# A fused attention and two feed-forward layers: v's first block by tokens, the constants as one row, smaller first loads

## The chip, the cores and the metric

The kernel runs on one core of a Trainium2 chip. Its engines are named as in the profile: PE (TensorE), DVE (VectorE), ACT (ScalarE), POOL (GpSimd) and SP (SyncE, which here only issues transfers). The metric is the device time of the kernel in microseconds (us); less is better.

## What is computed

Three stages in float32. The first is an attention over channels: the scores are a 256 x 256 matrix, and v is multiplied by their softmax.

```python
qn = q / (norm(q, axis=1) + 1e-6)                 # q, k, v: 6016 tokens x 256 channels
kn = k / (norm(k, axis=1) + 1e-6)
s = kn.T @ qn / tau
p = exp(s - s.max(-1));  p /= p.sum(-1) + 1e-9
x = v @ p                                          # 6016 x 256
h = x @ w_in                                       # 6016 x 2048
P = a[0] + a[1]*h + a[2]*h**2 + a[3]*h**3
Q = 1 + abs(b[0])*abs(h) + abs(b[1])*h**2
x = (P / (Q + 1e-6)) @ w_out                       # 6016 x 256
h = x @ w_in2
out = (h * clip(h + 3, 0, 6) / 6) @ w_out2         # 6016 x 256
```

## The kernel before, in words

Tokens are handled in tiles of 128 (47 of them, `TILES`), and behind the attention in blocks of four tiles (512 tokens; block 0 has three). C is 256 channels, F is 2048 hidden units, J = 16 chunks of 128 hidden units.

**Load stage.** q and k come in 24 loads (`loads`, line 65): tile 0 alone, then 23 pairs of tiles, in a ring of NQK = 8 buffers. SP issues them (lines 294 to 303), and from load 8 on it waits until the buffer has been multiplied by PE and squared by ACT. ACT issues k of load 0 itself (line 555). For each load PE adds k^T q into the PSUM tile OP (line 438; each product is four passes per tile), ACT squares q and k (line 574), and DVE adds the squares into square_sum (line 743). squares has two buffers, so ACT waits for DVE two loads back. Ahead of the first load PE runs `keep_clock(9)`, products of a matrix of ones.

**v and its transpose.** v is needed transposed. `load_v` (lines 285 to 292) brings a block in eight transfers, with runs of 32 channels (128 bytes), so that DVE's transpose of 32 x 32 squares (`v_transpose`, line 736) completes the transpose. For block 0 SP issues these eight after load 12 (`V0_LOADED`), and DVE transposes after load 14 (`V0_TRANSPOSED`). ACT rounds the result to the high half (`vT_split`, line 563), POOL subtracts for the low half (line 336). All products behind the attention take a high and a low half of each operand, as three passes (`split_product`, lines 405 to 407).

**Constants.** ACT issues three transfers that spread a, b and tau over all partitions (lines 556 to 558, 128 pieces each), and takes |b| and a square root of |b[1]| after load 2 (lines 576 to 580); DVE refines that root after load 3 (`exact_root`).

**Behind the loads.** After load 21 of 0 to 23 (`NORMS_BEHIND`) PE waits for `square_rows_summed` and sums the squares over the partitions (`norms`, line 419). ACT and DVE make inverse norms; PE spreads them after load 22 (`spread_inverse`, line 428). After load 23 DVE forms the logits (line 773), ACT their exponentials (line 594), PE transposes them (line 452). Then w_in1 is folded with them: `fold(n)` (line 465) gives two chunks of columns each, of which `fold_split` of ACT (line 604) and DVE (line 789) make halves; the first fold waits for the whole of w_in1 (line 454).

**Weights.** SP issues w_out1 in four parts (wd1), w_in1 in one transfer (line 306), v's block 1, w_in2 (wu2) and w_out2 (wd2) in four parts each. ACT rounds w_out1 (`wd1_round`, line 568) behind the loads, all four parts before the exponentials; POOL subtracts (`wd1_split`) once `square_rows_summed` is there; PE's `down1` waits for all four parts at its first chunk.

**Main part.** Step t has 16 slots j. In each slot, PE does `up2` and `down2` of the block before, `up1(t, j)`, and `down1` three chunks behind; ACT, DVE and POOL compute the gate functions in an order written out by hand in the `step` functions. In the first two steps, slots named in WU2_AT and WD2_AT also make the halves of w_in2 and w_out2. v's block t + 1 is transposed in slots 5 and 8. In step 0, `fold(n + 1)` comes behind `up1` of the chunk that uses fold n.

```python
LAG_DIVIDE = 1
LAG_DOWN1 = 3
...
V_AT = 5, 8
```

Of the kernel before, what the change touches and what calls it, by code (L numbers as in the profile page):

```python
# [26 lines left out]
P = 128  # L27


def attention_ffn_ffn(nc, q, k, v, tau, w_in1, w_out1, a, b, w_in2, w_out2, out):  # L30
# [25 lines left out]
    V0_LOADED, V0_TRANSPOSED = 12, 14  # L56

    NORMS_BEHIND, SPREAD_BEHIND = 21, 22
# [6 lines left out]
    loads = [(0, 1)] + [(i, min(QK, TILES - i)) for i in range(1, TILES, QK)]  # L65
    NQK = 8
    EPS_NORM, EPS_SUM, Q_CONST = 1e-6, 1e-9, 1.0 + 1e-6
# [3 lines left out]
    assert sum(PIECES) == J  # L71
# [17 lines left out]
    with ctx:  # L89
# [29 lines left out]
        v_blocks = sb("v_blocks", [P, CT, W], fp32)  # L119

# [34 lines left out]

        consts_in, qk_squared, qk_summed, qk_multiplied = map(
            sem, ("consts_in", "qk_squared", "qk_summed", "qk_multiplied"))
        qk_in = [sem(f"qk_in_{i}") for i in range(NQK)]
        w1_in, v_in = map(sem, ("w1_in", "v_in"))
# [111 lines left out]
        def _(sp):  # L271
# [3 lines left out]

            def load_wu2(part):
                half, c = part // 2, part % 2
                cols = slice(half * F // 2, (half + 1) * F // 2)
                sp.dma_start(wu2_raw[:, c, cols], w_up_h[1][:, c, cols]).then_inc(wu2_in[part], 16)
# [5 lines left out]
            def load_v(blk):  # L285
                m = width(blk) // P
                sp.wait_ge(vT_done, CT * blk)
                rows = tokens_of(v[0], blk, m).rearrange("(a q) (h b r) -> h b q a r", q=32, h=CT, b=4)
                to = v_blocks[:, :, 0:m * P].rearrange("p h (a r) -> p h a r", r=32)
                for c in range(CT):  # L290
                    for b in range(4):
                        sp.dma_start(to[32 * b:32 * (b + 1), c], rows[c, b]).then_inc(v_in, 16)

            for n, (i, m) in enumerate(loads):
                if n >= NQK:

                    sp.wait_ge(qk_multiplied, n - NQK + 1)
                    sp.wait_ge(qk_squared, n - NQK + 1)
                sp.dma_start(qk[:, n % NQK, 0, 0:m, :], q_h[:, i:i + m, :]).then_inc(qk_in[n % NQK], 16)
                if n >= 1:  # L300
                    sp.dma_start(qk[:, n % NQK, 1, 0:m, :], k_h[:, i:i + m, :]).then_inc(qk_in[n % NQK], 16)
                if n == V0_LOADED:
                    load_v(0)
            for part in range(4):
                load_wd1(part)
            sp.dma_start(w_raw_a[:], w_up_h[0]).then_inc(w1_in, 16)
            load_v(1)
            for part in range(4):
                load_wu2(part)
# [17 lines left out]
        def _(pool):  # L327
# [48 lines left out]
            for c in range(CT):  # L376
                vT_split(0, c, 0)

            pool.wait_ge(square_rows_summed, 1)
            for part in range(4):  # L380
                wd1_split(part)

            def step(t, par):
                for j in range(J):
                    if exists(t):
                        q_body(t, j)
                    if x := stage(t - 1, j - SHIFT2):
                        g2_split(*x)
                    if j in V_AT and exists(t) and exists(t + 1):
                        vT_split(t + 1, V_AT.index(j), 1 - par)  # L390
                    if slot(t, j) in WU2_AT:
                        wu2_split(WU2_AT.index(slot(t, j)))
                    if slot(t, j) in WD2_AT:
                        wd2_split(WD2_AT.index(slot(t, j)))
                    if y := stage(t, j - LAG_DIVIDE):
                        quotient_lo(*y)
# [5 lines left out]
        def _(pe):  # L402
# [30 lines left out]
            keep_clock(9)  # L433
            for n, (_, m) in enumerate(loads):
# [6 lines left out]
                done.then_inc(qk_multiplied, 1)  # L441
                if n == NORMS_BEHIND:
                    norms()
# [10 lines left out]
            pe.wait_ge(w1_in, 16)  # L454

            def fold(n):

                cols = columns(n)
                for c in range(CT):
# [23 lines left out]
            def down1(blk, j):  # L483
                w = width(blk)
                wait_chunk(pe, g1_lo_done, (blk, j))
                if j == 0 and isinstance(blk, int) and blk == 0:
                    pe.wait_ge(wd1_lo_done, 4)
# [64 lines left out]
        def _(act):  # L552

            _, m = loads[0]
            act.dma_start(qk[:, 0, 1, 0:m, :], k_h[:, 0:m, :]).then_inc(qk_in[0], 16)
            act.dma_start(coef[:, 0:4], a.partition_broadcast(P)).then_inc(consts_in, 16)
            act.dma_start(coef[:, 4:6], b.partition_broadcast(P)).then_inc(consts_in, 16)
            act.dma_start(coef[:, 6:7], tau.partition_broadcast(P)).then_inc(consts_in, 16)

            def vT_split(blk, c, par):  # L560
                w = width(blk)
                act.wait_ge(vT_done, CT * blk + c + 1)
# [7 lines left out]
            for n, (_, m) in enumerate(loads):  # L570
# [5 lines left out]
                if n == 2:  # L576
                    act.wait_ge(consts_in, 48)
# [3 lines left out]
                if n == V0_TRANSPOSED + 2:  # L581
                    for c in range(CT):
                        vT_split(0, c, 0)
# [6 lines left out]
            wd1_round(3)  # L590
# [90 lines left out]
            def step(t, par):  # L681
                for j in range(J):
# [15 lines left out]
                    if u2:  # L698
                        c2(*u2)
                    if slot(t, j) in WU2_AT:  # L700
                        wu2_round(WU2_AT.index(slot(t, j)))
# [9 lines left out]
        def _(dve):  # L711
# [18 lines left out]
            def v_transpose(blk, c, par):  # L730
                w = width(blk)
                if c == 0:
                    dve.wait_ge(v_in, 128 * (blk + 1))
# [5 lines left out]
            for n, (_, m) in enumerate(loads):  # L739
# [5 lines left out]
                if n == 3:  # L745
                    exact_root()
                if n == V0_TRANSPOSED:
                    for c in range(CT):
                        v_transpose(0, c, 0)
# [7 lines left out]
            dve.wait_ge(consts_in, 48)  # L757
# [135 lines left out]
```

## Time and profile before

| | us |
|---|---|
| runs shown (three) | 1155.82, 1157.50, 1157.81 |
| their median | 1157.5 |
| the profiled execution | 1158.11 |
| its span, first to last instruction | 1156.2 |
| PE busy in it | 1127.5 |
| DVE busy | 889.3 |
| ACT busy | 878.6 |
| POOL busy | 787.4 |

The span is the time between the first and the last instruction; the execution's own time is 1.9 us longer. The mean granted clock of PE is 0.992 of full speed. Busy times are sums over an engine's instructions. Four views are used below: the page, the chain of waits (from the last instruction back to what released each step), the instructions in order of time, with the idle time before each and what ended it in brackets, and stretches of fixed length with the busy time of each engine in them.

### The profile page before, as it was taken

How to read it: one execution, taken by the hardware profiler on the slowest of the kernel's cores; microseconds unless marked ns; L12 is line 12 of the kernel's file. 1: busy time of each engine (PE TensorE's matmuls, PEld its weight loads, DVE VectorE, ACT ScalarE, POOL GpSimd, SP SyncE). 2: the span in 40 equal slices, each digit the busy share in tenths (PEclk: the TensorE clock that was granted, in tenths of full speed). 3: DMA queues.
4: the chain of work that ended last, by engine and by line, in shares of the span. 5: the costliest groups of instructions: out<-in, count | busy, mean ns of one | idle time of the engine just before them, and what ended most of it. 6: DMA issues, size and time to landing. Idle time of an engine off the chain costs nothing.

```text
span 1156.2 us, 17900 instructions
## 1 busy us (share of the span) xinstructions
PE 1127.5 (98%) x6010; PEld 970.2 (84%) x6010; DVE 889.3 (77%) x1261; ACT 878.6 (76%) x1477; POOL 787.4 (68%) x628
## 2 busy tenths in 40 slices
PE   8988799999999999999999999999999999999998
PEld 7777588888888888888888888888888888888887
DVE  5679999887887887887787787787787788777621
ACT  5688888877877877777787787787787787787643
POOL 0458888776676676676676677677677677666643
PEclk9899899999999999999999999999999999999999
DMA  8951010010010010010010010010001000000000
GB/s 258 341 152 20 0 20 1 14 19 1 20 19 1 17 22 3 1 38 1 1 37 1 2 37 1 1 29 9 1 19 19 1 20 1 1 19 1 1 19 19
DMA packets 68378, 34.21 MB, mean 30 GB/s; under 512 B 51264, under 2 KB 61632, under 8 KB 68032
## 3 DMA queue, kind: packets, MB, share of 16 engines
q1 hardware_dynamic: 67712, 32.91, 10.3%
q8 instruction: 52, 0.85, 0.3%
q14 instruction: 38, 0.31, 0.1%
q10 hardware_dynamic: 576, 0.13, 0.1%
HBM read 26.87 MB, written 6.16 MB: 29 GB/s over the span
## 4 chain that ended last, share of the span: by engine, by line
PE 88%; DVE 6%; ACT 2%; issue 1%; DMA 1%; SPq 1%; POOL 0%; POOLq 0%; DVEq 0%; ACTq 0%
PE H L405 14%; PE H L406 14%; PE H L407 14%; PE OP L525 8%; PE OP L527 8%; PE OP L529 7%; PE YP L407 7%; PE YP L405 7%; PE YP L406 7%; DVE SQ L824 1%; DMA qk<-in_k 1%; PE OP L438 1%; DVE H L809 1%; DVE g_hi L817 1%; DVE square_sum L743 1%
## 5 line engine op out<-in xcount | busy, mean ns | idle before, releaser
L361 POOL TENSOR_TENSOR SQ<-SQ,AB 128x512 f32<-128x512 f32 (+1 forms) x192 | 248.0, 1292 | 283.4 <-ACT SQ L621 283.0
L373 POOL TENSOR_TENSOR g_lo<-R,g_hi 128x512 fp32r<-128x512 f32 (+1 forms) x192 | 245.1, 1276 | 30.6 <-ACT g_hi L652 30.6
L367 POOL TENSOR_TENSOR g_lo<-SQ,Y 128x512 fp32r<-128x512 f32 (+1 forms) x192 | 244.8, 1275 | 5.0 <-DVE SQ L832 5.0
L619 ACT ACTIVATE AB<-H,absb 128x512 f32<-128x512 f32 (+1 forms) x192 | 130.1, 678 | 151.2 <-PE H L407 150.0
L525 PE MATMUL OP<-wd_hi,g_hi 128*128 128x256 f32 x752 | 211.7, 282 | 0.6 <-POOL g_lo L373 0.6
L527 PE MATMUL OP<-wd_lo,g_hi 128*128 128x256 f32 x752 | 212.0, 282 | 0.0
L529 PE MATMUL OP<-wd_hi,g_lo 128*128 128x256 f32 x752 | 209.7, 279 | 0.0
L802 DVE TENSOR_TENSOR T<-T,H 128x512 f32<-128x512 f32 (+1 forms) x192 | 129.3, 674 | 103.9 <-ACT T L627 103.8
L817 DVE SCALAR_TENSOR_TENSOR g_hi<-H,coef,Y 128x512 fp32r<-128x512 f32 (+1 forms) x192 | 141.6, 738 | 68.3 <-ACT Y L640 67.3
L405 PE MATMUL H<-vT_hi,wf_hi 128*128 128x512 f32 (+1 forms) x384 | 151.3, 394 | 13.9 <-DVE wf_lo L789 8.1
L824 DVE SCALAR_TENSOR_TENSOR SQ<-SQ,g_hi 128x512 f32<-128x512 f32 (+1 forms) x192 | 155.4, 809 | 6.6
L646 ACT ACTIVATE R<-H 128x512 f32<-128x512 f32 (+1 forms) x192 | 113.2, 590 | 61.0 <-PE H L407 60.1
L838 DVE SCALAR_TENSOR_TENSOR R<-R,H 128x512 f32<-128x512 f32 (+1 forms) x192 | 128.2, 668 | 37.7 <-ACT R L646 37.7
L405 PE MATMUL YP<-g_hi,wd_hi 128*128 128x512 f32 (+1 forms) x384 | 151.5, 394 | 2.7 <-POOL g_lo L367 2.5
L405 PE MATMUL H<-yT_hi,wu_hi 128*128 128x512 f32 (+1 forms) x384 | 150.2, 391 | 0.7 <-issue 0.5
L406 PE MATMUL H<-vT_lo,wf_hi 128*128 128x512 f32 (+1 forms) x384 | 150.5, 392 | 0.0
L407 PE MATMUL H<-vT_hi,wf_lo 128*128 128x512 f32 (+1 forms) x384 | 150.4, 392 | 0.0
L407 PE MATMUL YP<-g_hi,wd_lo 128*128 128x512 f32 (+1 forms) x384 | 150.2, 391 | 0.0
L406 PE MATMUL H<-yT_lo,wu_hi 128*128 128x512 f32 (+1 forms) x384 | 149.7, 390 | 0.0
L406 PE MATMUL YP<-g_lo,wd_hi 128*128 128x512 f32 (+1 forms) x384 | 149.3, 389 | 0.0
L407 PE MATMUL H<-yT_hi,wu_lo 128*128 128x512 f32 (+1 forms) x384 | 149.0, 388 | 0.0
L525 PEld LDWEIGHTS OP<-wd_hi,g_hi 128*128 128x128 f32 x752 | 141.3, 188 | 8.8 <-POOL g_lo L373 0.8
(82 smaller groups left out, 2215.9 us busy)
## 6 DMA issues: line engine op xcount, KB each, us to landing
qk<-in_q SPq DMA_DIRECT2D x23, 256.0 KB, 5.4
qk<-in_k SPq DMA_DIRECT2D x23, 256.0 KB, 6.6
v_blocks<-in_v SPq DMA_DIRECT2D x88, 64.0 KB, 2.4
out<-o_tok SPq DMA_DIRECT2D x11, 512.0 KB, 3.0
wd_raw<-in_moe_w_out SPq DMA_DIRECT2D x8, 512.0 KB, 9.8
w_raw_a<-in_moe_w_in SPq DMA_DIRECT2D x1, 2048.0 KB, 13.6
wu_raw<-in_moe_w_in SPq DMA_DIRECT2D x4, 512.0 KB, 6.8
v_blocks<-in_v SPq DMA_DIRECT2D x8, 48.0 KB, 5.2
```

The source lines that it names most:

```text
L361: nc.gpsimd.tensor_tensor(SQ[:, j % 4, 0:w], SQ[:, j % 4, 0:w], AB[:, j % 2, 0:w], ALU.add)\
L367: nc.gpsimd.tensor_tensor(g1_lo[:, j % 4, 0:w], SQ[:, j % 4, 0:w], Y[:, j % 2, 0:w], ALU.mult)\
L373: nc.gpsimd.tensor_tensor(g2_lo[:, j % 4, 0:w], R[:, j % 2, 0:w], g2_hi[:, j % 4, 0:w].bitcast(fp32), ALU.subtract).then_inc(g2_lo_done, 1)
L405: nc.tensor.matmul(psum, w_hi, x_hi, start=first, stop=False)
L406: nc.tensor.matmul(psum, w_hi, x_lo, start=False, stop=False)
L407: return nc.tensor.matmul(psum, w_lo, x_hi, start=False, stop=last)
L525: nc.tensor.matmul(psum, g2_hi[:, j % 4, at], wd2_hi[:, j, :], start=first, stop=False, skip_group_check=True)
L527: nc.tensor.matmul(psum, g2_hi[:, j % 4, at], wd2_lo[:, j, :], start=False, stop=False, skip_group_check=True)
L529: done = nc.tensor.matmul(psum, g2_lo[:, j % 4, at], wd2_hi[:, j, :], start=False, stop=last, skip_group_check=True)
L619: nc.scalar.activation(AB[:, j % 2, 0:w], h, ACT.Abs, scale=absb[:, 0:1])
L817: nc.vector.scalar_tensor_tensor(g1_hi[:, j % 4, 0:w], h1(blk, j), A0, Y[:, j % 2, 0:w], ALU.add, ALU.mult).then_inc(g1_hi_done, 1)
L824: nc.vector.scalar_tensor_tensor(SQ[:, j % 4, 0:w], SQ[:, j % 4, 0:w], Q_CONST, g1_hi[:, j % 4, 0:w].bitcast(fp32), ALU.add, ALU.mult).the ...
```

## The change

- The first three tiles of q and k come as single loads, then 22 pairs: 25 loads. NORMS_BEHIND and SPREAD_BEHIND become 22 and 23, so they stand before the last two loads as they did. ACT issues k of loads 0 and 1. `keep_clock(9)` becomes `keep_clock(6)`.
- v's block 0 comes in one transfer, tokens on the partitions and 1 KB per token, after load 7. PE transposes it in six pieces after load 10, into the PSUM tile H; ACT copies the high halves and DVE subtracts for the low halves after load 14. POOL has no part in it.
- The constants come as one row on one partition, issued by ACT after its square of load 2. PE multiplies the row by a row of ones after load 6, which spreads it over the partitions; ACT copies it and takes |b| and the root after load 11, DVE refines the root after load 12.
- w_in1 comes in two halves of columns, behind parts 1 and 2 of w_out1; w_out1's part 3, w_in2's part 0 and v's block 1 follow. `fold` waits for the half that it needs.
- w_out1's part 3 is rounded and subtracted in slot 0 of step 0, and `down1` waits for each part where it needs it.

```diff
@@ settings @@
-    V0_LOADED, V0_TRANSPOSED = 12, 14
-    NORMS_BEHIND, SPREAD_BEHIND = 21, 22
+    V0_LOADED, V0_TRANSPOSED, V0_SPLIT = 7, 10, 14
+    COEF_SPREAD, COEF_USED = 6, 11
-    loads = [(0, 1)] + [(i, min(QK, TILES - i)) for i in range(1, TILES, QK)]
+    SINGLE = 3
+    loads = [(i, 1) for i in range(SINGLE)] + [(i, min(QK, TILES - i)) for i in range(SINGLE, TILES, QK)]
+    NORMS_BEHIND, SPREAD_BEHIND = len(loads) - 3, len(loads) - 2
@@ SP @@
+            def load_w1(half):
+                cols = slice(half * F // 2, (half + 1) * F // 2)
+                sp.dma_start(w_raw_a[:, :, cols], w_up_h[0][:, :, cols]).then_inc(w1_in[half], 16)
             def load_v(blk):
-                sp.wait_ge(vT_done, CT * blk)
+                if exists(blk - 2):
+                    sp.wait_ge(vT_done, CT * (blk - 1))
+                else:
+                    sp.wait_ge(vT_psum, CT)
...
-                if n >= 1:
+                if n >= 2:
                     sp.dma_start(qk[:, n % NQK, 1, 0:m, :], k_h[:, i:i + m, :]).then_inc(qk_in[n % NQK], 16)
                 if n == V0_LOADED:
-                    load_v(0)
-            for part in range(4):
-                load_wd1(part)
-            sp.dma_start(w_raw_a[:], w_up_h[0]).then_inc(w1_in, 16)
+                    m = tiles_of[0]
+                    sp.dma_start(v_tok[:, 0:m, :], tokens_of(v[0], 0, m).rearrange("(i p) c -> p i c", p=P))\
+                      .then_inc(v0_in, 16)
+            load_wd1(0)
+            load_wd1(1)
+            load_w1(0)
+            load_wd1(2)
+            load_w1(1)
+            load_wd1(3)
+            load_wu2(0)
             load_v(1)
-            for part in range(4):
+            for part in range(1, 4):
                 load_wu2(part)
@@ POOL @@
-            for c in range(CT):
-                vT_split(0, c, 0)
             pool.wait_ge(square_rows_summed, 1)
-            for part in range(4):
+            for part in range(3):
                 wd1_split(part)
...
+                    if slot(t, j) == 0:
+                        wd1_split(3)
@@ PE @@
-            keep_clock(9)
+            keep_clock(6)
...
+                if n == COEF_SPREAD:
+                    pe.wait_ge(consts_in, 48)
+                    nc.tensor.matmul(YP[:, 1, 0:7], ones[0:1, :], coef_row[:, 0:7], start=True, stop=True)\
+                      .then_inc(consts_spread, 1)
+                if n == V0_TRANSPOSED:
+                    pe.wait_ge(ident_ready, 1)
+                    pe.wait_ge(v0_in, 16)
+                    for c in range(CT):
+                        for i in range(tiles_of[0]):
+                            done = nc.tensor.transpose(H[:, c, i * P:(i + 1) * P], v_tok[:, i, c * P:(c + 1) * P],
+                                                       ident[:])
+                        done.then_inc(vT_psum, 1)
...
-            pe.wait_ge(w1_in, 16)
+                if PIECE_AT[n] in (0, J // 2):
+                    pe.wait_ge(w1_in[PIECE_AT[n] // (J // 2)], 16)
...
-                if j == 0 and isinstance(blk, int) and blk == 0:
-                    pe.wait_ge(wd1_lo_done, 4)
+                if j % 4 == 0 and isinstance(blk, int) and blk == 0:
+                    pe.wait_ge(wd1_lo_done, j // 4 + 1)
@@ ACT @@
-            _, m = loads[0]
-            act.dma_start(qk[:, 0, 1, 0:m, :], k_h[:, 0:m, :]).then_inc(qk_in[0], 16)
-            act.dma_start(coef[:, 0:4], a.partition_broadcast(P)).then_inc(consts_in, 16)
-            act.dma_start(coef[:, 4:6], b.partition_broadcast(P)).then_inc(consts_in, 16)
-            act.dma_start(coef[:, 6:7], tau.partition_broadcast(P)).then_inc(consts_in, 16)
+            for n, (i, m) in enumerate(loads[:2]):
+                act.dma_start(qk[:, n, 1, 0:m, :], k_h[:, i:i + m, :]).then_inc(qk_in[n], 16)
...
                 if n == 2:
-                    act.wait_ge(consts_in, 48)
+                    act.dma_start(coef_row[:, 0:4], a.rearrange("(o n) -> o n", o=1)).then_inc(consts_in, 16)
+                    act.dma_start(coef_row[:, 4:6], b.rearrange("(o n) -> o n", o=1)).then_inc(consts_in, 16)
+                    act.dma_start(coef_row[:, 6:7], tau.rearrange("(o n) -> o n", o=1)).then_inc(consts_in, 16)
+                if n == COEF_USED:
+                    act.wait_ge(consts_spread, 1)
+                    nc.scalar.activation(coef[:, 0:7], YP[:, 1, 0:7], ACT.Copy).then_inc(consts_ready, 1)
+                    act.wait_ge(consts_ready, 1)
                     nc.scalar.activation(absb[:], coef[:, 4:6], ACT.Abs).then_inc(absb_ready, 1)
...
-                if n == V0_TRANSPOSED + 2:
+                if n == V0_SPLIT:
+                    w = width(0)
                     for c in range(CT):
-                        vT_split(0, c, 0)
+                        act.wait_ge(vT_psum, c + 1)
+                        nc.scalar.activation(vT_hi[0][:, c, 0:w], H[:, c, 0:w], ACT.Copy).then_inc(vT_hi_done, 1)
...
-            wd1_round(3)
...
+                    if slot(t, j) == 0:
+                        wd1_round(3)
@@ DVE @@
-                if n == 3:
+                if n == COEF_USED + 1:
                     exact_root()
-                if n == V0_TRANSPOSED:
+                if n == V0_SPLIT:
+                    w = width(0)
                     for c in range(CT):
-                        v_transpose(0, c, 0)
+                        dve.wait_ge(vT_hi_done, c + 1)
+                        nc.vector.tensor_tensor(vT_lo[0][:, c, 0:w], H[:, c, 0:w], vT_hi[0][:, c, 0:w].bitcast(fp32),
+                                                ALU.subtract).then_inc(vT_lo_done, 1)
```

## Rows read from the trace of the kernel before

**Rows 1.** The page: busy time by engine, and the chain that ended last, by engine.

```profile
PE 1127.5 (98%) x6010; PEld 970.2 (84%) x6010; DVE 889.3 (77%) x1261; ACT 878.6 (76%) x1477; POOL 787.4 (68%) x628
...
PE 88%; DVE 6%; ACT 2%; issue 1%; DMA 1%; SPq 1%; POOL 0%; POOLq 0%; DVEq 0%; ACTq 0%
```

**Rows 2.** The chain of waits, 0 to 64 us (start us, us, what).

```profile
1.67 7.17 DMA qk<-in_k
...
47.60 0.70 DVE square_sum L751
...
50.22 3.62 PE OP L438 x8
53.84 0.85 PE YP L428 x4
...
56.72 0.50 DVE o_tok L773
```

**Rows 3.** Stretches of 1 us: busy of PE, PEld, DVE, ACT, POOL; PEclk, DMA share, GB/s.

```profile
18.00:19.00 1.00, 1.00 (x7) 0.87 (x6) 0.90 (x2) 0.73 (x2) 0.00 (x0) 1.00 1.06 395
...
24.00:25.00 1.00, 1.00 (x7) 0.87 (x6) 1.00 (x1) 1.00 (x1) 0.00 (x0) 1.00 0.47 69
...
48.00:49.00 1.00, 0.65 (x3) 0.65 (x4) 0.29 (x1) 0.20 (x1) 0.63 (x1) 0.56 1.18 413
...
55.00:56.00 1.00, 1.00 (x6) 0.89 (x5) 0.22 (x1) 0.00 (x0) 1.00 (x2) 1.00 0.65 66
```

**Rows 4.** In order of time, 0 to 30 us (start us, us, engine, line; [idle before]).

```profile
5.00 1.91 PE L438 MATMUL OP<-qk 128*128 128x256 f32 x4
...
8.89 21.35 PE L438 MATMUL OP<-qk 128*128 128x256 f32 x97 [1.97 <-DMA qk<-in_k]
...
10.48 1.06 ACT L574 ACTIVATE squares<-qk 128x1024 f32<-128x1024 f32 x1 [0.56 <-DMA qk<-in_k]
...
11.65 1.28 ACT L580 ACT_TABLE_LOAD   x1
...
16.94 8.57 SPq L292 DMA_DIRECT2D v_blocks<-in_v  x8
...
18.63 1.06 ACT L574 ACTIVATE squares<-qk 128x1024 f32<-128x1024 f32 x1 [0.27 <-DVE square_sum L743]
```

**Rows 5.** In order of time, 29 to 60 us, the same columns.

```profile
29.73 1.06 ACT L574 ACTIVATE squares<-qk 128x1024 f32<-128x1024 f32 x1 [3.40 <-DMA qk<-in_k]
29.75 15.91 PE L438 MATMUL OP<-qk 128*128 128x256 f32 x72
...
37.50 10.06 DVE L743 TENSOR_TENSOR square_sum<-square_sum,squares 128x1024 f32<-128x1024 f32 x7 [0.47 <-ACT squares L574]
...
45.97 2.23 ACT L568 ACTIVATE wd_hi<-wd_raw 128x1024 fp32r<-128x1024 f32 x2
...
48.35 1.87 PE L419 MATMUL YP<-ones,square_sum 128*128 128x1 f32 x8 [2.68 <-DVE square_sum L751]
48.37 9.28 POOL L336 TENSOR_TENSOR wd_lo<-wd_raw,wd_hi 128x1024 fp32r<-128x1024 f32 x4 [8.54 <-DVE square_sum L751]
...
56.45 1.50 PE L413 MATMUL H<-ones 128*128 128x128 f32 x12
```

**Rows 6.** DMA queues and issues, 0 to 12 us (KB each, us to landing).

```profile
q10 hardware_dynamic: 576, 0.13, 5.2%
...
coef<-in_tau ACTq DMA_DIRECT2D x1, 0.5 KB, 7.8
```

**Rows 7.** In order of time, DVE and POOL in the first slots.

```profile
65.05 0.56 DVE L802 TENSOR_TENSOR T<-T,H 128x384 f32<-128x384 f32 x1 [2.66 <-ACT T L627]
...
67.67 1.35 POOL L361 TENSOR_TENSOR SQ<-SQ,AB 128x384 f32<-128x384 f32 x1 [2.20 <-ACT SQ L621]
```

**Rows 8.** Stretches of 10 us and of 2 us, columns as in rows 3.

```profile
70.00:80.00 10.00, 8.02 (x43) 7.20 (x41) 9.29 (x18) 9.27 (x21) 7.29 (x7) 1.00 0.30 96
...
124.00:126.00 2.00, 0.00 (x0) 0.00 (x0) 1.88 (x3) 1.87 (x4) 1.95 (x3) 0.50 0.00 0
```

More of the change, by code:

```diff
@@ L70, in attention_ffn_ffn @@
     PIECE_AT = [sum(PIECES[:i]) for i in range(len(PIECES))]
-    assert sum(PIECES) == J
+    assert sum(PIECES) == J and J // 2 in PIECE_AT
     QUARTER, UNIT = J * C // 4, J * C // 8
@@ L119, in attention_ffn_ffn @@
         v_blocks = sb("v_blocks", [P, CT, W], fp32)
+        v_tok = v_blocks[:].rearrange("p h w -> p (h w)").rearrange("p (i c) -> p i c", c=C)
+        coef_row = sb("coef_row", [1, 8], fp32)
         o_tok = sb("o_tok", [P, BT, C], fp32)
@@ L153, in attention_ffn_ffn @@
         A0, A1, A2, A3, B0, B1, TAU = (coef[:, i:i + 1] for i in range(7))
+        consts_ready = sem("consts_ready")
         consts_in, qk_squared, qk_summed, qk_multiplied = map(
@@ L158, in attention_ffn_ffn @@
         qk_in = [sem(f"qk_in_{i}") for i in range(NQK)]
-        w1_in, v_in = map(sem, ("w1_in", "v_in"))
+        w1_in = [sem(f"w1_in_{i}") for i in range(2)]
+        v0_in, v_in, vT_psum, consts_spread = map(sem, ("v0_in", "v_in", "vT_psum", "consts_spread"))
         wd1_in, wu2_in, wd2_in = ([sem(f"{x}_in_{i}") for i in range(4)] for x in ("wd1", "wu2", "wd2"))
@@ L552, in _ @@
         def _(act):
-            _, m = loads[0]
-            act.dma_start(qk[:, 0, 1, 0:m, :], k_h[:, 0:m, :]).then_inc(qk_in[0], 16)
-            act.dma_start(coef[:, 0:4], a.partition_broadcast(P)).then_inc(consts_in, 16)
-            act.dma_start(coef[:, 4:6], b.partition_broadcast(P)).then_inc(consts_in, 16)
-            act.dma_start(coef[:, 6:7], tau.partition_broadcast(P)).then_inc(consts_in, 16)
+            for n, (i, m) in enumerate(loads[:2]):
+                act.dma_start(qk[:, n, 1, 0:m, :], k_h[:, i:i + m, :]).then_inc(qk_in[n], 16)
             def vT_split(blk, c, par):
                 w = width(blk)
-                act.wait_ge(vT_done, CT * blk + c + 1)
+                act.wait_ge(vT_done, CT * (blk - 1) + c + 1)
                 nc.scalar.activation(vT_hi[par][:, c, 0:w], vT_raw[par][:, c, 0:w], ACT.Copy).then_inc(vT_hi_done, 1)
@@ L732, in v_transpose @@
                 if c == 0:
-                    dve.wait_ge(v_in, 128 * (blk + 1))
+                    dve.wait_ge(v_in, 128 * blk)
                     if exists(blk - 2):
@@ L756, in _ @@
             ratio, norm, norm_k = small[:, 12:16], YP[:, 0, 8:12], small[:, 16:18]
-            dve.wait_ge(consts_in, 48)
+            dve.wait_ge(consts_ready, 1)
             dve.wait_ge(roots_taken, 1)
```

## The prediction

> **What bounds the kernel now.** I read the page first: PE is busy 98% of the span and carries 88% of the chain that ended last [rows 1]. From about 140 us on, time is matmul time, which this change does not touch. What can be won lies in the start, where an earlier finish moves everything behind it one for one. So I read the start in the chain of waits, then in stretches of 1 us, then in order of time.
>
> PE computes the product of k and q until 45.7 us and then waits for DVE's sum of squares: the fold of its two halves starts at 47.60 [rows 2], the norms' matmuls at 48.35, after 2.68 us of idle PE [rows 5]. Then come norms, load 22, the spread of the inverses and load 23, until DVE takes the logits at 56.72 [rows 2]. The granted clock falls at 48 and is back at 1.00 by 55 [rows 3]; between, PE runs at 1.2 of 2.4 GHz, and load 22 took 3.62 us [rows 2] for what takes 1.73 at full clock.
>
> Why is DVE late? Eight v issues (L292) hold SP for 8.57 us from 16.94 [rows 4]. DMA falls from 395 to 69 GB/s [rows 3], and ACT and DVE run dry near 27 us: the wait of ACT that ends at 29.73 took 3.40 us [rows 5]. Otherwise DVE is the pace: 7 adds in 10.06 us [rows 5] include waits, and where nothing is late ACT starts a square each 1.33 us, 1.06 of work and 0.27 of waiting for DVE [rows 4]. PE hardly notices the hole (its passes run on from 8.89 to 45.66, broken off only near 29.75): those 42 tiles in 36.8 us [rows 4, 5], allowing 0.5 for gaps, give 0.863 per tile, 1.73 per pair, more than a pair's 1.33 on DMA or DVE. PE is the slowest of the three in the load stage, yet DVE comes last.
>
> **The change, part by part.**
>
> *Start of the load stage.* Tile 0 runs from 5.00 to 6.91 at 0.48 us a pass, half speed, then PE idles 1.97 until the pair of tiles 1 and 2 has landed; the next pair came at 10.48 [rows 4]. With single tiles and 12 warm-up passes instead of 18, tile 0 starts near 3.9 and tiles 1 and 2 fit into the wait. After that PE needs load 3 (tiles 3 and 4, the old load 2). Bounds for it: 10.45 as now, and 7.6, when PE would be through with tiles 0 to 2 at full speed. The constants' packets (most of the 576 on ACT's queue; tau took 7.8 us to land [rows 6]) lie among the first tiles and now go as three short rows. I take 9.4, nearer the old row, as the queue still starts slowly. Load 1's k now goes by ACT's queue. It landed 7.17 us after its issue began [rows 2], and an issue is under 0.5, so issuing is not what was late. The Trainium skill, "DMA: Bandwidth & Descriptors", section "Issuing engines are not separate DMA queues", says that a second issuing engine saves only the time of issuing. By it the pair would come at most 0.5 us sooner, 9.95, and the total gain would be 0.55 smaller; the range holds that.
>
> *v's first block.* SP's eight issues become one of about 0.45 us for 384 KB, 1.0 us of DMA at 390 GB/s. PE gets six 128x128 transposes: 0.75 at the warm-up's pace of 12 passes in 1.50 [rows 5], 1.3 at the pace of the 4 passes of the spread, 0.85 [rows 2]; I take 1.0, between. PE now waits for v at load 10, with all later matmuls behind it. It is issued after load 7, near 12 us; with even 7.2 us to land it is there by 20, PE at 9.4 + 8 x 1.73 = 23: no wait. POOL loses two subtractions that nobody waited for: 0. DVE loses its two transposes and gets two subtractions of 0.56 (its 128x384 form from PSUM [rows 7]), 1.15 with waits; ACT copies ahead of it.
>
> *Constants.* 0.2 us of PE behind load 6 (there at 16.3). ACT issues the rows after its third square, near 8 us, three at 0.45, before load 3 is needed. If the last took 7.8 us as now it lands by 17.3: 0 to 1 us of PE wait; I take 0, since a single row is less than 128. The work on them (copy, abs, table load 1.28 [rows 4], root: 1.75 us) moves from load 2 to load 11, where ACT leads DVE by only 0.27 + 0.24: DVE starves 1.24 us, plus 0.78 for the exact root that it computes.
>
> *DVE's new end.* Squares of load 3 done at 10.5; 22 pairs at 1.33, 29.3; 1.24 + 0.78 + 1.15; fold 0.7: 43.7. *PE's new end of load 22*: 9.4 + 20 x 1.73 + 1.0 + 0.2 = 45.2. So PE no longer waits: norms at 45.3 instead of 48.35. SP must wait for PE before load 24 (buffer of load 16 free at 35); it lands by 41, ahead of both.
>
> *Behind the sum.* PE arrives without an idle stretch, so I let the clock stay up: norms 1.0 (1.87 at half [rows 5]), pair 1.73, spread 0.5, pair 1.73, hand-over 0.1: logits at 50.4 instead of 56.72, **6.3 us sooner**. The inverses take ACT and DVE 1.5 us, inside the pair's 1.73. On ACT, rounds 0 and 1 of w_out1 (landed by 42) are done by 46, round 2 and the exp table by 50. w_in1's first half lands near 45, its second near 49, and the first fold comes at 53: halving it gives 0 here, costs 0.5 us of SP.
>
> *What is given back.* Round 3 of w_out1 (half of 2.23 [rows 5], 1.0 us) moves from an idle ACT into slot 0, ahead of the next root; POOL's part (a quarter of 9.28 [rows 5]) falls where POOL idled 2.20 for ACT [rows 7]. ACT has no gap there, so its 1.0 is lost whole, plus 0 to 1 from POOL running beside DVE; I take **1.2**. The split wait on w_out1: 0, all parts were there. v block 1 is issued about 2 us earlier and needed at slot 5: 0. w_in2's first part lands before slot 2: 0.
>
> **Sum:** -6.3 + 1.2 = -5.1 us. The profiled execution took 1158.1 (span 1156.2), so 1153.0; the median of the three runs shown, 1157.5, gives 1152.4. I say 1152.6, between, as the three differ by 2.0 among themselves.
>
> **The rivals.**
> (a) *The sum of squares is late again.* For: two stalls of ACT and DVE now lie in steady state, and adds at 1.33 never catch up. Against: the v hole (3.4) goes, and DVE leads by 1.5. Ready at 46.5, it costs 1.2: 1153.8. Ready at 48, the clock falls as it did, and only some 0.4 of the stage and none of its low clock is won; with 1.2 given back, 1158.3, no change. Between them 1156. Chance 0.09.
> (b) *The clock falls in the first slots*, where PE idles 1 us more. PE was busy 8.02 of 10 us from 70 to 80 at clock 1.00 [rows 8]; at half clock that is 16, so 10 us of it do the work of 6.2 and cost 3.8: 1156.4, no change. For: the clock was 0.50 at 124 to 126, where PE stood still [rows 8]. Against: idle stretches between slots are one us, not five. Chance 0.06.
> (c) *Slower: PE stays at half clock in the load stage.* Six fewer warm-up passes, and waits between single tiles. Each pair so run costs 1.73 more and nothing hides it, since PE is the pace. Three pairs cancel the gain; from 4.3 (until about 24 us) it is slower by over 0.2%; six give 1163.0. For: half speed lasted from the first pass to past 6.9. Against: at 8.89, after 1.97 us of waiting, it was gone [rows 4], and the waits are now shorter. The Trainium skill, "TensorE: Matmul & The Clock Gate", section "What's actually happening", says that throttled is the default and activity releases it; by that, less warm-up speaks for this rival. Tiles 1 and 2 replace it, however. Chance 0.04.
> (d) *The change does not do what it says*: DMA thins out after load 7 for a reason other than SP's eight issues. DVE then ends near 46.7, PE waits 1.5: 1154.1. Chance 0.05.
> Forecast: 0.76.
>
> **How the numbers follow.** 0.2% is 2.3 us, about what a measurement of this kernel can tell from no change, so faster means below 1155.2. Forecast, (d) and a third of (a) are faster; the rest of (a) and (b) no change; (c) slower: 0.84, 0.12, 0.04. Bounds of the terms: load 3 at 7.6 leaves DVE's 43.7 to decide, -1.5; slot 0 without loss, -1.2; load 3 as now +1.05, constants late +1, POOL +0.8, and PE's low clock near 124 may last 0.5 longer or shorter. Not all at once: 1150.2 to 1155.8, with (d) and the mild (a) inside.
>
> **What would show it.** Right: no thin DMA at 22 to 28; PE without a gap from load 3 to the norms, whose wait for square_sum is gone; clock 1.00 from 45 to 60; logits near 50.4; a slot 1 about 1 us later against slot 0. Wrong: PE waits for constants or v; a clock of 0.5 before 60; a pair at 3.4 us after 8 us; norms still near 48.

## The result, and the profile after

The changed kernel takes 1141.47 us (median of four runs, 1141.41 to 1142.12), the kernel before 1157.51 (1155.82 to 1157.81): the ratio is 0.9866, with a 95% interval of 0.9849 to 0.9883. Forecast were 1152.6, at most 1155.8 and at least 1150.2. The sign was right, the gain was 16.0 us instead of 4.9, and the range missed it by 9 us.

The page after (busy time by engine; the chain by engine), beside [rows 1]:

```profile
PE 1112.6 (98%) x6012; PEld 960.9 (84%) x6012; DVE 889.3 (78%) x1262; ACT 878.9 (77%) x1479; POOL 782.6 (69%) x626
...
PE 91%; DVE 5%; ACT 2%; issue 1%; DMA 0%; POOL 0%; SPq 0%; POOLq 0%; DVEq 0%; ACTq 0%
```

PE is busy for 14.9 us less, though it has two passes more to do. Up to the logits it is busy for 51.6 us before and 47.6 after; most of that is the low clock behind the loads. From the first output copy to the end it has 5032 instructions in both kernels and is busy for 928.4 us before and 918.2 after. These 10.2 us are new; the prediction has no term for them.

The chain of waits at the start (start us, us, what), beside [rows 2]:

```profile
8.19 7.17 PE OP L459 x32
...
44.15 0.79 PE YP L440 x8
44.94 1.83 PE OP L459 x8
46.77 0.48 PE YP L449 x4
...
49.09 0.49 DVE o_tok L816
```

The wait for square_sum is gone from the chain. PE goes from the loads straight into the norms; the load behind the norms takes 1.83 us instead of 3.62, and DVE has the logits at 49.09 instead of 56.72. Stretches of 1 us (length, busy of PE, PEld, DVE, ACT, POOL; PEclk, DMA share, GB/s), beside [rows 3]:

```profile
24.00:25.00 1.00, 1.00 (x7) 0.87 (x6) 1.00 (x1) 0.85 (x1) 0.00 (x0) 1.00 1.05 383
...
48.00:49.00 1.00, 1.00 (x7) 0.90 (x6) 0.00 (x0) 0.98 (x2) 0.45 (x1) 1.00 1.09 380
55.00:56.00 1.00, 1.00 (x6) 0.95 (x6) 0.00 (x0) 0.99 (x3) 0.00 (x0) 1.00 0.67 106
```

DMA moves 383 GB/s at 24 us where it moved 69, and the clock stays at 1.00. In order of time, beside [rows 4]:

```profile
3.76 2.23 PE L459 MATMUL OP<-qk 128*128 128x256 f32 x8
...
6.36 1.13 PE L459 MATMUL OP<-qk 128*128 128x256 f32 x4 [0.36 <-DMA qk<-in_k]
...
7.96 0.51 SPq L319 DMA_DIRECT2D v_blocks<-in_v  x1
8.16 1.06 ACT L605 ACTIVATE squares<-qk 128x1024 f32<-128x1024 f32 x1 [1.20 <-DMA qk<-in_k]
...
22.61 0.82 PE L472 MATMUL H<-ident,v_blocks 128*128 128x128 f32 x6
```

v goes out in one issue of 0.51 us. Tiles 3 and 4 have landed at 8.16 instead of 10.48. The six transposes take 0.66 us of PE by the chain. Behind the loads, beside [rows 5, 7]:

```profile
42.41 0.69 DVE L794 TENSOR_TENSOR square_sum<-square_sum 128x512 f32<-128x512 f32 x1
...
43.99 0.95 PE L440 MATMUL YP<-ones,square_sum 128*128 128x1 f32 x8
...
55.71 0.58 ACT L657 ACTIVATE AB<-H,absb 128x384 f32<-128x384 f32 x1
...
57.20 1.07 ACT L599 ACTIVATE wd_hi<-wd_raw 128x1024 fp32r<-128x1024 f32 x1
...
58.35 2.39 POOL L357 TENSOR_TENSOR wd_lo<-wd_raw,wd_hi 128x1024 fp32r<-128x1024 f32 x1 [0.50 <-ACT wd_hi L599]
...
59.87 0.56 ACT L657 ACTIVATE AB<-H,absb 128x384 f32<-128x384 f32 x1
```

DVE's fold starts at 42.41 and the norms at 43.99, about 0.9 us after it ends. Round 3 of w_out1 sits in slot 0 (57.20), POOL's part behind it (58.35). From AB of slot 0 to AB of slot 1 it is 4.16 us; it was 63.34 to 66.55, 3.21. So the start keeps 7.63 - 0.95, some 6.7 us. ACT's copy of the first block's output starts at 215.71 instead of 222.08: 6.4 us sooner.

**Where the other 10 us are.** The spans differ by 16.6 us (1156.2 and 1139.6), so 10.2 come behind the first output. The copies of the later blocks drift apart, block by block. ACT's copies of two successive outputs, before and then after:

```profile
849.79 1.01 ACT L667 ACTIVATE o_tok<-OP 128x1024 f32<-128x1024 f32 x1
...
939.29 1.01 ACT L667 ACTIVATE o_tok<-OP 128x1024 f32<-128x1024 f32 x1
```

```profile
836.23 1.01 ACT L705 ACTIVATE o_tok<-OP 128x1024 f32<-128x1024 f32 x1
...
924.77 1.01 ACT L705 ACTIVATE o_tok<-OP 128x1024 f32<-128x1024 f32 x1
```

A block takes 89.50 us before and 88.54 after; between most of its neighbours it is the same to 0.02 us. Yet PE is never idle there, and its clock is 1.00 in both (20 us of each, columns as above, before and then after):

```profile
900.00:920.00 20.00, 20.00 (x106) 16.98 (x105) 14.87 (x21) 14.80 (x26) 12.91 (x11) 1.00 0.00 1
```

```profile
900.00:920.00 20.00, 20.00 (x112) 17.28 (x112) 16.50 (x24) 15.92 (x28) 14.79 (x12) 1.00 0.01 1
```

PE's own instructions start at shorter distances. The profile models the end of a matmul, so the starts are compared. The first of the twelve passes of the second down product in a slot, and the instruction behind the twelve, before and after:

```profile
903.84 0.28 PE L525 MATMUL OP<-wd_hi,g_hi 128*128 128x256 f32 x1
...
905.26 0.40 PE L405 MATMUL H<-vT_hi,wf_hi 128*128 128x512 f32 x1
```

```profile
900.75 0.28 PE L559 MATMUL OP<-wd_hi,g_hi 128*128 128x256 f32 x1
...
902.12 0.40 PE L426 MATMUL H<-vT_hi,wf_hi 128*128 128x512 f32 x1
```

Twelve passes take 1.42 us before and 1.37 after. Over three whole blocks, the passes of the second down product follow each other every 118.3 ns before and 114.7 after, and the 512-column passes every 231.9 and 230.9. With 192 and 288 of them in a block that is 0.68 + 0.28 = 0.96 us. The passes of the loop are the same. What differs is that the new tensor coef_row (its declaration is not in the cut diff above) takes 32 bytes per partition behind v_blocks, so o_tok, yT, R, g2, T, SQ, AB, Y and g1 lie 32 bytes further on, while weights and v lie where they were.

### The profile page after: what moved, and what is told of

The parts are those of the page before. It is cut to its first block, busy times and chain, and to the rows that moved or that the text cites. A ratio compares the mean times of both kernels' runs of the same rounds, so it can differ in the third digit from the quotient of the medians.

```text
span 1139.6 us, 17909 instructions
## 1 busy us (share of the span) xinstructions
PE 1112.6 (98%) x6012; PEld 960.9 (84%) x6012; DVE 889.3 (78%) x1262; ACT 878.9 (77%) x1479; POOL 782.6 (69%) x626
## 3 DMA queue, kind: packets, MB, share of 16 engines
q1 hardware_dynamic: 65328, 32.78, 10.2%
## 4 chain that ended last, share of the span: by engine, by line
PE 91%; DVE 5%; ACT 2%; issue 1%; DMA 0%; POOL 0%; SPq 0%; POOLq 0%; DVEq 0%; ACTq 0%
PE H L426 15%; PE H L428 14%; PE H L427 14%; PE OP L559 7%; PE OP L563 7%; PE OP L561 7%; PE YP L426 7%; PE YP L428 7%; PE YP L427 7%; PE OP L459 3%; DVE SQ L867 1%; DVE H L852 1%; DVE g_hi L860 1%; DVE T L845 1%; DMA qk<-in_k 0%
## 5 line engine op out<-in xcount | busy, mean ns | idle before, releaser
L559 PE MATMUL OP<-wd_hi,g_hi 128*128 128x256 f32 x752 | 209.2, 278 | 0.6 <-POOL g_lo L394 0.6
L563 PE MATMUL OP<-wd_hi,g_lo 128*128 128x256 f32 x752 | 209.0, 278 | 0.0
L561 PE MATMUL OP<-wd_lo,g_hi 128*128 128x256 f32 x752 | 208.9, 278 | 0.0
L852 DVE SCALAR_TENSOR_TENSOR H<-T,coef,H 128x512 f32<-128x512 f32 (+1 forms) x192 | 143.0, 745 | 6.7
L561 PEld LDWEIGHTS OP<-wd_lo,g_hi 128*128 128x128 f32 x752 | 141.2, 188 | 8.2
```

The source lines that it names most:

```text
L559: nc.tensor.matmul(psum, g2_hi[:, j % 4, at], wd2_hi[:, j, :], start=first, stop=False, skip_group_check=True)
L561: nc.tensor.matmul(psum, g2_hi[:, j % 4, at], wd2_lo[:, j, :], start=False, stop=False, skip_group_check=True)
L563: done = nc.tensor.matmul(psum, g2_lo[:, j % 4, at], wd2_hi[:, j, :], start=False, stop=last, skip_group_check=True)
L852: nc.vector.scalar_tensor_tensor(h, T[:, j % 2, 0:w], A1, h, ALU.add, ALU.mult).then_inc(t3_done, 1)
```

## The experiments

Eighteen kernels ran. Block times are the distance of ACT's output copies in the second half of the loop; for the kernels with a single run the block time is what is read. Each ratio is to the kernel before, on the same chip, with its 95% interval. The chip is not the same for all experiments, and the kernel before had medians of 1157.3 to 1159.0 us on them.

**The shift alone, and the change without it.** pad32 is the kernel before with an unused tensor; row_in_small is the changed kernel with the row in spare columns.

```diff
 v_blocks = sb("v_blocks", [P, CT, W], fp32)
+sb("pad", [P, 8], fp32)                        # pad32
...
-coef_row = sb("coef_row", [1, 8], fp32)
+coef_row = small[0:1, 41:48]                   # row_in_small
```

> The kernel before, with one unused tensor of 32 bytes per partition behind v_blocks and nothing else, so that o_tok, yT, R, g2, T, SQ, AB, Y and g1 lie where they lie in the changed kernel (yT_hi at byte 158144 instead of 158112, a multiple of 64). The changed kernel's blocks in the long loop take 88.53 us each, those of before 89.49, with PE never idle in either. Theory A (where the tensors lie sets PE's pace): 88.5 us a block and about 1147 us in all, the start as before (logits at 56.7). Rival B (the program, its waits or the start set the pace): 89.5 a block and 1157.5.

> The changed kernel, with the row of constants in seven unused columns of the tensor small, so that no tensor is moved against the kernel before. Theory A: blocks of 89.5 us, about 1152 us in all, the start as in the changed kernel (logits at 49.1). Rival B: 88.5 us a block and 1141.5.

pad32: 1146.77 us, ratio 0.9897 (0.9873 to 0.9920), with this pair of copies, 88.53 us apart:

```profile
841.68 1.01 ACT L668 ACTIVATE o_tok<-OP 128x1024 f32<-128x1024 f32 x1
...
930.21 1.01 ACT L668 ACTIVATE o_tok<-OP 128x1024 f32<-128x1024 f32 x1
```

row_in_small: 1151.81 us, ratio 0.9943 (0.9924 to 0.9961), blocks of 89.49, logits at 48.56. The kernel before had a median of 1158.2 us on that chip. Theory A holds in both directions: 32 unused bytes are worth 11.4 us by themselves, and the change without them is worth 6.4, which is inside the forecast. The logits of pad32 came at 55.66, where 56.7 was expected; the paragraph on place or distance shows why.

**Other distances.** The same padding with 64, 96, 160, 480 and 544 bytes.

> The kernel before with 64 unused bytes at the same place: the tensors move, but they start 32 bytes past a multiple of 64 as before. Theory A in its sharp form (the remainder by 64 decides): 89.5 us a block and 1157.5. If the address matters in another way (the distance between tensors before and behind the padding, or a larger unit), anything between 88.5 and 90 a block.

> The kernel before with 96 unused bytes at the same place: yT_hi at byte 158208, a multiple of 128. Sharp form of theory A (remainder by 64): as with 32 bytes, 88.5 us a block and 1147. If the remainder by 128 also counts (the changed kernel's is 64), it is faster than with 32 bytes.

> The kernel before with 160 unused bytes behind v_blocks: the back is at remainder 64 by 128 again, but 128 bytes further than with 32. If the pattern repeats every 128 bytes: 88.5 us a block and 1147. If it is longer than 128 or no pattern of this kind at all: another block time, 89.5 or more.

> The kernel before with 544 = 512 + 32 unused bytes behind v_blocks. With 32 the blocks take 88.53 us, with 160 = 128 + 32 they take 89.60. If the pattern of places repeats with 512 bytes (or 256): 88.53 a block. If not, 89.5 or more, and what counts is no remainder by a small power of two.

> The kernel before with 480 unused bytes behind v_blocks, by 512 the step of 32 bytes to the other side. No theory of mine gives the number: 88.5 us a block would say that several places are fast, 89.5 or more that the fast one stands alone among the six tried.

| bytes behind v_blocks | block, us | kernel, us | ratio (95%) |
|---|---|---|---|
| 0 (before) | 89.49 | 1157.5 | |
| 32 | 88.53 | 1146.8 | 0.9897 (0.9873 to 0.9920) |
| 64 | 89.60 | 1159.0 | 1.0008 (0.9995 to 1.0020) |
| 96 | 89.81 | 1159.6 | 1.0010 (0.9998 to 1.0022) |
| 160 | 89.60 | 1158.6 | 0.9999 (0.9989 to 1.0009) |
| 480 | 88.64 | 1147.9 | one run |
| 544 | 88.53 | 1148.1 | one run |

The copies with 96 bytes, 89.81 apart:

```profile
850.52 1.01 ACT L668 ACTIVATE o_tok<-OP 128x1024 f32<-128x1024 f32 x1
...
940.33 1.01 ACT L668 ACTIVATE o_tok<-OP 128x1024 f32<-128x1024 f32 x1
```

The sharp form of theory A fell: with 96 bytes the tensors start at a multiple of 64, and of 128, and their blocks are longer than before. A pattern of 128 fell with 160 bytes. 544 = 512 + 32 gives the block time of 32, so a pattern of 512 (or 256) fits. 480 is a second fast place, with another mix of passes (119 ns for the second down product, 226 to 227 for the 512-column passes that read yT or g1).

**Place or distance.** both_moved puts 64 bytes in front of all tensors and 32 behind v_blocks; all_moved puts 32 in front of all and none behind.

```diff
+sb("pad_a", [P, 16], fp32)    # both_moved; [P, 8] in all_moved
 wf_hi, wf_lo = (sb(f"wf_{x}", [P, CT, F], f32r) for x in ("hi", "lo"))
...
 v_blocks = sb("v_blocks", [P, CT, W], fp32)
+sb("pad_b", [P, 8], fp32)     # both_moved alone
```

> Remainders by 128 of the start bytes, in the four kernels so far: weights and v (in front) 0; yT, R, g2, T, SQ, AB, Y, g1 (behind) 32, 64, 96 and 0 for 0, 32, 64 and 96 bytes of padding, and only 64 was fast. Here 64 unused bytes stand in front of all and 32 behind v_blocks: the front lies at 64 and the back at 0. Theory A1 (what counts is how front and back lie to each other, 64 apart is fast): 88.5 us a block, 1147. Theory A2 (the place of the back tensors alone counts): as with 96 bytes, whose back lies at the very same bytes, 89.8 a block and 1159.

> The kernel before with 32 unused bytes in front of all tensors: the back at the very bytes of the fast kernels, but the front (weights, v) moved as well. Theory A1 (how front and back lie to each other): 89.49 us a block. Theory A2 (the place of the back itself): 88.53.

both_moved: blocks of 88.53, 1144.66 us, ratio 0.9882 (0.9863 to 0.9902), with its back tensors at the very bytes at which pad96 is slow. all_moved: blocks of 89.49, 1158.5 us in its one run, with its back tensors at the bytes of the fast kernels. So the place itself does not decide. The distance between what lies in front (weights, v) and behind (yT, g2, g1) does.

both_moved is also 2 us ahead of pad32 at the start: its logits come at 53.65 instead of 55.66. Most of that is the granted clock, as the norms start at 48.45 and 48.81. The stretch of 2 us behind the norms, both_moved and then pad32 (columns as above):

```profile
50.00:52.00 2.00, 2.00 (x13) 1.70 (x12) 1.21 (x8) 1.98 (x3) 2.00 (x2) 1.00 1.02 434
```

```profile
50.00:52.00 2.00, 2.00 (x6) 1.60 (x6) 1.29 (x8) 1.98 (x4) 2.00 (x2) 0.53 0.98 410
```

Thirteen of the profiled kernels have the start of the kernel before. Behind the idle time in front of the norms the clock was at half for about 7 us in five of them (the kernel before is one), for about 3.5 us in seven, and not at all in both_moved; their logits came between 53.65 and 58.17. The start of a single profile can therefore not be compared to a microsecond, while block times at equal distances agree within 0.02 us.

**Whose tensors.** Two trials, g2_only and all_but_g2, were made before the pattern was known. They restored places by steps of 128 bytes, which pad160 shows not to be neutral.

```diff
+sb("pad_a", [P, 8], fp32)     # g2_only; [P, 24] in all_but_g2, with [P, 8] behind v_blocks
 g2_hi, g2_lo = (sb(f"g2_{x}", [P, 4, W], f32r) for x in ("hi", "lo"))
+sb("pad_b", [P, 24], fp32)    # [P, 8] in all_but_g2
```

> The kernel before with 32 unused bytes in front of g2_hi and 96 behind g2_lo: g2 (the stationary operand of the second down product) alone stands at remainder 64, the rest of the back at 32 as before. The passes that have g2 start every 118.2 ns before and every 114.7 in the changed kernel; 192 of them a block are 0.67 of the 0.96 us. Theory A3 (the place of g2 itself counts for them): 114.7 ns, 88.8 us a block, near 1151. Rival (they are slow through traffic of the other engines on R, T, SQ, AB and Y): 118 ns and 1158.

> The counterpart: 32 bytes behind v_blocks, 96 in front of g2_hi, 32 behind g2_lo, so that all of the back but g2 stands at remainder 64 and g2 at 32. Theory A3: g2's passes at 118 ns, 89.2 us a block, near 1155. Rival (the other engines' tensors count): 114.7 ns and near 1149.

Blocks of 89.60 and 89.71; 1157.61 and 1158.63 us, ratios 0.9999 (0.9986 to 1.0011) and 1.0005 (0.9993 to 1.0018). Since g1 stood 128 and 160 bytes off in them, they say nothing of g2 alone. With steps of 480 and 32 bytes, 512 together, the test is cleaner:

> The kernel before with unused bytes (32, 480, 32, 480, 32) in front of yT, R, g2, T and g1: the tensors of the back that PE reads (yT, g2, g1) stand 32 bytes further by 512, as in the fast kernels, and R, T, SQ, AB and Y where they stood. Theory P (PE's own reads set its pace): 88.53 us a block, 1147. Theory E (the other engines' traffic does): 89.49 a block, 1157.

> The counterpart: R, T, SQ, AB and Y 32 bytes further by 512, yT, g2 and g1 where they stood. Theory P: 89.49 us a block. Theory E: 88.53.

Their copies, pe_tensors and then other_tensors:

```profile
842.17 1.01 ACT L672 ACTIVATE o_tok<-OP 128x1024 f32<-128x1024 f32 x1
...
930.70 1.01 ACT L672 ACTIVATE o_tok<-OP 128x1024 f32<-128x1024 f32 x1
```

```profile
851.44 1.01 ACT L671 ACTIVATE o_tok<-OP 128x1024 f32<-128x1024 f32 x1
...
940.93 1.01 ACT L671 ACTIVATE o_tok<-OP 128x1024 f32<-128x1024 f32 x1
```

88.53 against 89.49, and 1147.5 against 1159.7 us in one run each. Theory P holds as far as it was put: where the tensors stand that PE reads sets its pace, and this shift of the tensors that only the other engines use does not. One rival is not separated by it. yT, g2 and g1 are written by ACT, DVE and POOL, and these writes moved with PE's reads, so that it is PE's own reads that meet is argued and not shown. That R, T, SQ, AB and Y stood 512 and 1024 bytes off in pe_tensors is taken as neutral from pad544.

**v's first block.** Only v's loading, transposing and splitting go back (L292, L736, L563 and L336 of the kernel before), with the issue after load 13.

```diff
-    V0_LOADED, V0_TRANSPOSED, V0_SPLIT = 7, 10, 14
+    V0_LOADED, V0_TRANSPOSED = 13, 15
```

> The changed kernel with v's first block as before: eight transfers of 128-byte runs after load 13 (tiles 23 and 24, the same point in the data), DVE transposing after load 15, POOL subtracting. No tensor is moved. Theory (v's eight issues starve ACT and DVE, DVE's sum comes late, PE idles and its clock falls): thin DMA for about 7 us, norms at 47 to 49, the granted clock at 0.5 behind them, logits near 56 instead of 49.1, 1141.5 + 6.5 = 1148. Rival (the single first tiles and the constants bring the gain): norms near 44.5, no fall of the clock, 1142 to 1143.

1147.10 us, ratio 0.9907 (0.9888 to 0.9925). PE's norms and the load behind them, one microsecond of the thin DMA (39 GB/s; it was under 240 from 20 to 26 us), and the granted clock behind the norms:

```profile
46.57 1.05 PE L437 MATMUL YP<-ones,square_sum 128*128 128x1 f32 x8 [2.94 <-DVE square_sum L778]
47.49 3.06 PE L456 MATMUL OP<-qk 128*128 128x256 f32 x8
```

```profile
23.00:24.00 1.00, 1.00 (x7) 0.87 (x6) 0.93 (x4) 0.38 (x1) 0.00 (x0) 1.00 0.25 39
50.00:52.00 2.00, 2.00 (x9) 1.79 (x8) 0.43 (x1) 1.17 (x1) 2.00 (x2) 0.59 1.08 373
52.00:54.00 2.00, 2.00 (x15) 1.84 (x14) 0.55 (x2) 0.00 (x0) 1.55 (x1) 1.00 1.17 282
```

The wait for square_sum is back (2.94 us), the load takes 3.06, the logits come at 53.4 instead of 49.1. That is the theory's mechanism; at the logits it costs 4.3 us for the 7 expected, in all 5.6 for 6.5. The clock was back at 1.00 by 52 here, after some 3.5 us at half, where it had stayed low from 48 to 55 in the kernel before; about 3.4 us less at half clock are 1.7 us by estimate, the larger part of what is missing.

**The first loads.** Tile 0 and then pairs, nine warm-up products.

```diff
-    SINGLE = 3
+    SINGLE = 1
-                if n >= 2:        # k by SP
+                if n >= 1:
-            keep_clock(6)
+            keep_clock(9)
-            for n, (i, m) in enumerate(loads[:2]):
+            for n, (i, m) in enumerate(loads[:1]):
```

> The changed kernel with the first loads as before: tile 0 alone, then pairs (24 loads), load 1's k issued by SP, nine warm-up products. No tensor is moved. Theory (PE is the pace of the load stage, so only its start counts): norms about 1 us later, since the pair of tiles 1 and 2 lands near 8 and tiles 3 and 4 follow without a gap: 1142.5. Rival (the singles bring most of the 3 us by which norms come earlier): norms at 46.5 to 47, 1144.

1140.43 us, ratio 0.9846 (0.9828 to 0.9865), against 0.9866 for the changed kernel. The totals overlap, and the traces do not order them either. By the start of the norms' matmuls, the kernels with pairs have 43.47 (loads_old) and 43.91 (joined, below), those with single loads 43.99 (the changed kernel), 43.46 (row_in_small) and 43.84 (round3_early, below); the logits come at 48.57 and 49.01, and at 49.09, 48.56 and 48.94. In loads_old the pair of tiles 1 and 2 has landed at 5.81 and PE has hardly a gap:

```profile
4.63 1.03 PE L459 MATMUL OP<-qk 128*128 128x256 f32 x4
5.83 8.37 PE L459 MATMUL OP<-qk 128*128 128x256 f32 x37 [0.17 <-DMA qk<-in_k]
```

Theory and rival both expected a loss, of 1 and of 2.5 us. None is seen: the single loads bring nothing that can be told once the pair lands so early.

**The constants**, on loads_old, as they were before. The row, its product on PE and the later work on it are gone.

```diff
-                if n == COEF_SPREAD:
...
+            act.dma_start(coef[:, 0:4], a.partition_broadcast(P)).then_inc(consts_in, 16)
+            act.dma_start(coef[:, 4:6], b.partition_broadcast(P)).then_inc(consts_in, 16)
+            act.dma_start(coef[:, 6:7], tau.partition_broadcast(P)).then_inc(consts_in, 16)
```

> The kernel loads_old (first loads as before) with the constants as before too: three spreads over 128 partitions issued by ACT at the start, the work on them after load 2. In loads_old the pair of tiles 1 and 2 landed at 5.8 us, in the kernel before at 8.8. Theory (the constants' small pieces delay the first tiles): 8.4 to 8.9 us again, norms 2 to 3 us later than in loads_old (43.6), about 1142.5 to 1143.5. Rival (it was chance or the shorter queue): 6 us, norms at 43.6, and DVE two stalls better off, 1140.

1142.44 us, ratio 0.9861 (0.9833 to 0.9890), norms at 45.76, logits at 50.85:

```profile
5.00 1.91 PE L459 MATMUL OP<-qk 128*128 128x256 f32 x4
8.46 5.73 PE L459 MATMUL OP<-qk 128*128 128x256 f32 x24 [1.54 <-DMA qk<-in_k]
```

The same pair is awaited until 8.46 instead of 5.83, and tile 0 takes 1.91 us for 1.03. The theory holds, 2.3 us at the norms (45.76 for 43.47). The other profiles say the same: ACT could start on the pair at 7.54 to 9.33 in the fourteen kernels with the three spreads at the start, and at 5.81 and 6.20 in the two that have the pair without them.

**Round 3 of w_out1.** Behind the exponentials instead of in slot 0, with POOL's subtraction behind the other three.

```diff
                 .then_inc(exp_summed, 1)
+            wd1_round(3)
...
-                    if slot(t, j) == 0:
-                        wd1_round(3)
```

> The changed kernel with round 3 of w_out1 on ACT taken out of slot 0 and put behind the exponentials, where ACT waits 1.2 us for PE's first fold, and POOL's subtraction of it put behind the other three. No tensor is moved. Theory (the round in slot 0 costs 0.9 us, as slot 1 shows against slot 0): slot 1 comes 0.9 us sooner, 1140.6. Rival (that time is given back before PE is the bound, or the round is late behind the fold): 1141.5 or more.

1140.84 us, ratio 0.9853 (0.9835 to 0.9871). AB of slots 0 and 1 are 3.22 us apart, as before the change:

```profile
55.56 0.58 ACT L656 ACTIVATE AB<-H,absb 128x384 f32<-128x384 f32 x1
...
58.78 0.56 ACT L656 ACTIVATE AB<-H,absb 128x384 f32<-128x384 f32 x1
```

The 0.95 us are really there. At the first output copy this kernel is 0.82 us ahead (214.89 for 215.71), of which 0.15 were there at slot 0 already, and the medians differ by 0.6, less than the intervals can tell.

**Both together.**

> The changed kernel with the first loads as before (tile 0, then pairs, nine warm-up products) and with round 3 of w_out1 behind the exponentials. Places as in the changed kernel. If the two gains at the start add up (logits 0.5 us earlier, slot 1 another 0.9 earlier): 1139.8 to 1140.2, blocks of 88.53. If the fall of the clock between steps 0 and 1 eats one of them: 1140.5 to 1141.5.

1140.38 us, ratio 0.9855 (0.9838 to 0.9871): nothing gained over loads_old. Part 3 of w_out1 landed late in this run, and ACT waited for it in front of the first fold:

```profile
52.55 1.06 ACT L597 ACTIVATE wd_hi<-wd_raw 128x1024 fp32r<-128x1024 f32 x1 [0.89 <-DMA wd_raw<-in_moe_w_out]
```

The AB of slot 0 came at 56.02, 0.8 us later than in loads_old (55.19), and that of slot 1 only 0.1 us sooner (59.24 for 59.35). Then the granted clock fell in the first slots:

```profile
68.00:70.00 2.00, 2.00 (x6) 1.57 (x5) 1.74 (x4) 1.33 (x4) 1.59 (x2) 0.50 0.28 91
```

In loads_old it did not, and its first output copy came 0.5 us sooner (214.33 for 214.82).

## Why the prediction was right and wrong

- **The step that failed** is in the first paragraph of the prediction: that the time from 140 us on "is matmul time, which this change does not touch". It took the passes' pace for a constant of the work, and a change of it at nothing. The change added a tensor, the tensor moved PE's operands by 32 bytes, and the pace rose by 1.1%: a block takes 88.53 us instead of 89.49, and pad32, with these 32 bytes alone, is 11.4 us faster. Behind the first output that is 10.2 us, the difference between the 6.4 won there and the 16.6 between the spans. None of the rivals had it, so nothing in the range could.
- **The start was right.** Without the shift the change gives 1151.81 us; 1152.6 was forecast, 1150.2 to 1155.8 the range. Its mechanism is seen in all six profiles that have v's new transfer: no wait for square_sum, and no fall of the clock before the first slots. How much it wins depends on the execution it is compared with. The profile before had its logits at 56.72, near the middle of the 53.65 to 58.17 of the thirteen with the old start, so the 7.6 us at the logits is neither the best nor the worst case.
- *Start of the load stage*: the bound of 7.6 was nearer than the 9.4 taken; load 3 had landed at 8.16 (7.40 to 8.02 in the three other profiles with the same first loads). The reason given first, the constants' packets, was right and taken too small: they held the pair back by 2.6 us. The single loads, given as the way to fill the wait, fill a wait that is no longer there. ACT's queue brought nothing to be seen, as expected: the norms start at 43.46 to 43.99 with k of load 1 issued by ACT, and at 43.47 and 43.91 with it issued by SP. The Trainium skill, "DMA: Bandwidth & Descriptors", section "Issuing engines are not separate DMA queues", agrees with that. The 9.95 that was worked out by it took the landing of load 3 as in the kernel before, and the light constants moved that landing.
- *v's first block*: right. Transposes 0.66 us for 1.0, no wait of PE, thin DMA gone.
- *Constants*: 0.31 us of PE for 0.2, no wait for their landing. DVE's last fold ended at 43.1 for 43.7.
- *Behind the sum*: 5.10 us from the norms to the logits for 5.06. The clock stayed up. Logits at 49.09 for 50.4, nearly all of it from load 3's landing.
- *Given back*: 0.95 us in slot 0 for 1.2. POOL cost nothing to be seen.
- Rivals (a) to (d) did not come in the changed kernel. The fall of (b) came in two kernels with the new load stage or most of it, joined and constants_old (clock 0.50 near 69 us). It lasted about 3.5 us, and joined lost 0.6 us against loads_old between slot 1 and the first output, not the 3.8 worked out. As to (c), tile 0 took 1.03 us in loads_old and 1.91 in constants_old, behind the same nine warm-up products; what raised the clock sooner in the first is open.

## What to carry to other kernels

Where an engine is busy all the time, ask what sets the time of one of its instructions, not only how many there are. Any edit that adds or resizes a tensor moves everything allocated behind it: compare a new kernel with one that has only the padding before you credit the edit, and try a few paddings between a matmul's operands, by steps of 32 bytes. Of the six tried here, three (32, 480 and 544 bytes) won 9 to 11 us and three (64, 96 and 160) won nothing; no other kernel was tried. A few hundred tiny transfer pieces at the start can hold back the first large tiles by microseconds.

## What the runs showed of the hardware

- PE's pace with no idle time and full clock depends on where its operands lie in SBUF: 88.53 to 89.81 us a block over seven distances, 1.4%. Front and back moved together change nothing (89.49 twice); 512 bytes more change nothing (88.53 twice); 128 bytes more do (88.53 and 89.60). The tensors that only DVE, ACT and POOL use did not matter for it, in the one shift tried.
- The pace belongs to the whole sequence of passes and not to one pass: all types of pass shift with the padding, some of them up when the block gets shorter. With 480 bytes the second down product is no faster than before (119 ns) and the passes on yT and g1 are (226 to 227 ns, for 227 to 234). Passes whose operands did not move change too: vT_hi with wf_lo goes from 236 to 227 or 228 ns with 32 bytes. The places are not the whole rule either: from the second last to the last output copy, where only the passes of the last block are left, pad32 and loads_old take 42.4 us and the changed kernel 43.05, with the operands at the same places. What collides, and whether anything does, was not found; which of yT, g2 and g1 matters was not tried cleanly.
- Three spreads of 16, 8 and 4 bytes to 128 partitions, issued in the first 3 us, held the next 512 KB back from 5.8 to 8.4 us.
- In the thirteen kernels with the old start, PE's idle time in front of the norms was followed by about 7 us at half clock in five profiles, 3.5 in seven and none in one; the logits came between 53.65 and 58.17 us. In the five kernels that have the new load stage whole (the changed one, row_in_small, round3_early) or with the old first loads (loads_old, joined), PE did not idle there, the clock stayed at 1.00, and the logits came within 0.6 us of each other (48.56 to 49.09).
